# Recurrent attention and two feed-forward layers: staged loads, spare matmuls before the first tile, a new order of the first levels

## What is computed

```python
# r, k, v, w: [4, 8, 768, 48], u: [8, 48]
state = 0
for t in range(768):
    cur = einsum('bhd,bhe->bhde', u * k[t], v[t])
    y[t] = einsum('bhd,bhde->bhe', r[t], state + cur)
    state = w[t][..., None] * state + einsum('bhd,bhe->bhde', k[t], v[t])
x = y as [3072, 384]
h = x @ w_in                          # 384 x 2048
g = where(h >= 1, h, where(h <= -1, 0, (h + 1)**2 / 4))
x = g @ w_out                         # 2048 x 384
h = x @ w2_in
g = where(h > 0, h, exp(min(h, 0)) - 1)
out = g @ w2_out
```

## Time and profile before

| | us |
|---|---|
| median of 3 runs | 1023.39 (1021.88 to 1026.11) |
| the profiled execution | 1023.31 |
| its span in the profile | 1021.5 |
| TensorE (PE) busy | 989.6 (97%) |
| VectorE (DVE) busy | 554.2 (54%) |
| ScalarE (ACT) busy | 517.4 (51%) |
| GpSimd (POOL) busy | 46.7 (5%), all of it in the first 80 us |

### The profile page before, as it was taken

The page is one execution under the profiler, slowest core; times in us unless marked ns, Lnnn a source line. Parts: engine busy times, 40 slices in busy tenths (PEclk is TensorE's granted clock), DMA queues, the critical chain, the costliest instruction groups (busy, mean ns, idle before and its releaser), DMA issues.

```text
span 1021.5 us, 25102 instructions
## 1 busy us (share of the span) xinstructions
PE 989.6 (97%) x11080; PEld 812.3 (80%) x11080; DVE 554.2 (54%) x824; ACT 517.4 (51%) x926; POOL 46.7 (5%) x44
## 2 busy tenths in 40 slices
PE   4799899999999999999999999999999999999998
PEld 4788888777777777787778888888888888888886
DVE  5687877667666766776643454433433333333332
ACT  3465356454635354545456775554445444444543
POOL 5830000000000000000000000000000000000000
PEclk9899999999999999999999999999999999999999
DMA  9622032032002203020206000000000001000000
GB/s 327 200 79 96 24 121 110 3 141 78 33 28 115 80 33 115 28 80 33 95 1 216 1 31 31 32 21 11 32 31 1 31 32 31 31 1 1 31 1 31
DMA packets 24699, 61.71 MB, mean 60 GB/s; under 512 B 2448, under 2 KB 6928, under 8 KB 24592
## 3 DMA queue, kind: packets, MB, share of 16 engines
q1 hardware_dynamic: 24592, 60.12, 16.7%
HBM read 50.68 MB, written 9.44 MB: 59 GB/s over the span
## 4 chain that ended last, share of the span: by engine, by line
PE 90%; DVE 4%; POOL 2%; issue 1%; ACT 1%; DMA 1%; SPq 0%; ACTq 0%; DVEq 0%; POOLq 0%
PE down_banks L576 39%; PE up_bank L576 29%; PE g_banks L576 17%; PE y_bank L576 3%; DVE att L1025 1%; POOL win_lo L515 1%; PE y_bank L628 1%; DMA scratch<-w_in_dram 1%; PE y_bank L710 1%; POOL r_nat L525 0%; DVE r_nat L1054 0%; DVE att L1007 0%; DVE att L1037 0%; DVE ynat L1075 0%; DVE ynat L1078 0%
## 5 line engine op out<-in xcount | busy, mean ns | idle before, releaser
L576 PE MATMUL down_banks<-g_hi,wout_lo 128*128 128x512 f32 (+1 forms) x624 | 246.1, 394 | 0.0
L576 PE MATMUL down_banks<-g_hi,wout_hi 128*128 128x512 f32 (+1 forms) x624 | 235.9, 378 | 0.0
L576 PE MATMUL down_banks<-g_lo,wout_hi 128*128 128x512 f32 (+1 forms) x624 | 235.5, 377 | 0.0
L821 ACT CAST g_hi<-scratch 128x512 fp32r<-128x512 f32 (+1 forms) x192 | 116.0, 604 | 188.8 <-PE down_banks L576 118.9
L1096 DVE TENSOR_TENSOR g_lo<-scratch,g_hi 128x512 fp32r<-128x512 f32 (+1 forms) x192 | 128.4, 669 | 108.6 <-ACT g_hi L821 107.0
L576 PE MATMUL up_bank<-x_hi,win_lo 128*128 128x512 f32 (+1 forms) x480 | 182.6, 380 | 3.0 <-DVE g_lo L1096 1.8
L576 PE MATMUL up_bank<-x_lo,win_hi 128*128 128x512 f32 (+1 forms) x480 | 179.5, 374 | 0.0
L576 PE MATMUL up_bank<-x_hi,win_hi 128*128 128x512 f32 (+1 forms) x480 | 179.4, 374 | 0.0
L576 PEld LDWEIGHTS down_banks<-g_hi,wout_lo 128*128 128x128 f32 x624 | 117.8, 189 | 23.6
L576 PEld LDWEIGHTS down_banks<-g_hi,wout_hi 128*128 128x128 f32 x624 | 117.9, 189 | 23.3
L576 PEld LDWEIGHTS g_banks<-att 64*64 64x64 f32 (+1 forms) x5184 | 105.5, 136 | 36.2 <-issue 20.5
(11 more groups left out here) (98 smaller groups left out, 1075.6 us busy)
## 6 DMA issues: line engine op xcount, KB each, us to landing
att<-rT_dram SPq DMA_DIRECT2D x12, 512.0 KB, 4.0
att<-kT_dram SPq DMA_DIRECT2D x12, 512.0 KB, 5.6
att<-wT_dram SPq DMA_DIRECT2D x12, 512.0 KB, 6.5
r_nat<-rN_dram SPq DMA_DIRECT2D x12, 384.0 KB, 6.7
k_nat<-kN_dram SPq DMA_DIRECT2D x12, 384.0 KB, 7.7
att<-vN_dram SPq DMA_DIRECT2D x12, 384.0 KB, 6.9
x_dram<-r_nat SPq DMA_DIRECT2D x18, 256.0 KB, 2.3
ynat<-x_dram SPq DMA_DIRECT2D x6, 768.0 KB, 4.3
```

The lines of the kernel that those rows point to most:

```text
L576: return nc.tensor.matmul(out, lhsT, rhs, start=start, stop=stop, **kw)
L821: return nc.scalar.copy(out, in_)
```

## The change

- **Loads.** SP's first list is cut up by waits: a load is issued when an earlier one has landed (`landed(i)` waits for piece i). The order changes too: pieces 9 to 12 come before group 1's r, k and w, the others behind. Pieces 6 to 13 get buffers of their own (`extra`, `outer`), so their waits in `STAGED_BEHIND` go. The room comes from `dynamic_dma_scratch_size=2048`.
- **Spare matmuls.** `keep_busy(n)` issues n matmuls of 128x128 by 128x512 on zeros (a slice of `x_lo[1]` that DVE clears first) into `up_bank[1]`, which nothing reads: 9 before level 0, 5 after each of the levels 0 to 5, 3 after the last, and 2, 2 and 4 around the turns of x.
- **DVE.** In chunk 0, group 0 the next decays come before the mask. The mask of level 0 is for every chunk and group a product with a mask of ones and zeros (a `tensor_tensor` that writes all odd columns) in place of a predicated copy.
- **ACT.** A copy of one column at the very start has the function table loaded there. Pieces 9 to 12 are rounded where 9 to 16 were; 13 and 14 behind the rounding of x and the copy of k, the others two at a time in slots 0 to 2.
- **POOL.** Low parts 0 to 2, keys and bonus of group 0, low parts 3 to 5, the clearing of `near[1]`, low part 6, the product with v of group 0 (which no longer waits for low part 8), keys of group 1, low parts 7 to 18.
- **Diagonal.** ("values", 1, 1) moves from slot 19 to slot 21.

```diff
-                  16: [("sums", 1, 0), ("values", 1, 0)], 18: [("bonus", 1, 1), ("sums", 1, 1)], 19: [("values", 1, 1)],
+                  16: [("sums", 1, 0), ("values", 1, 0)], 18: [("bonus", 1, 1), ("sums", 1, 1)], 21: [("values", 1, 1)],
...
-STAGED_BEHIND = {**{i: 5 for i in range(9, 14)}, 18: 2, 19: 8, 20: 8, 22: 16, 23: 17, 24: 18, 25: 22, 26: 23, 27: 21}
-IDLE_PIECES = 9, 17
-PIECES_OF_SLOT = {0: (17, 18), **{f: (18 + f,) for f in range(1, 10)}}
+STAGED_BEHIND = {18: 2, 22: 16, 23: 17, 24: 18, 25: 22, 26: 23, 27: 21}
+IDLE_PIECES = 9, 13
+IDLE_AFTER_LEVEL = (5, 5, 5, 5, 5, 5, 3)
+PIECES_OF_SLOT = {0: (15, 16), 1: (17, 18), 2: (19, 20), **{f: (18 + f,) for f in range(3, 10)}}
...
             load_channels(0)
             load(masks_d, masks[:, :, :].rearrange("p l t -> p (l t)"), masks_in)
-            load_pieces(range(0, 3))
-            load_natural(0, 0)
+            load_pieces(range(0, 2))
+            sp.wait_ge(rk_in[0], 32)
+            load_pieces(range(2, 3))
+            load_natural_r(0, 0)
+            sp.wait_ge(w_in[0], 16)
+            load_natural_k(0, 0)
+            landed(0)
             load(uN, u_nat[:, :], bonus_in)
-            load_pieces(range(3, 6))
+            load_pieces(range(3, 4))
+            landed(1)
+            load_pieces(range(4, 5))
+            landed(2)
+            load_pieces(range(5, 6))
+            sp.wait_ge(nat_in[0], 32)
             load(vN[0, 0], v_[0], v_in[0])
-            load_natural(0, 1)
-            load_pieces(range(6, 9))
+            load_natural_r(0, 1)
+            landed(3)
+            load_natural_k(0, 1)
+            landed(4)
+            load_pieces(range(6, 7))
+            landed(5)
+            load_pieces(range(7, 8))
+            sp.wait_ge(v_in[0], 16)
+            load_pieces(range(8, 9))
             load(ident_d, ident[:, :], ident_in)
-            load_pieces(range(14, 19))
-            load_pieces(range(9, 14))
-            load_channels(1)
-            load_pieces(range(19, 21))
+            sp.wait_ge(nat_in[1], 32)
+            load_pieces(range(9, 12))
+            landed(6)
+            load_pieces(range(12, 13))
+            landed(7)
+            load(rT[0, 1], r_[1], rk_in[1])
+            landed(8)
+            load(kT[0, 1], k_[1], rk_in[1])
+            landed(9)
+            landed(10)
+            load(wT[0, 1], w_[1], w_in[1])
+            landed(11)
+            landed(12)
+            load_pieces(range(13, 15))
+            sp.wait_ge(rk_in[1], 32)
+            load_pieces(range(15, 17))
+            sp.wait_ge(w_in[1], 16)
+            load_pieces(range(17, 21))
...
-                pool.wait_ge(w1_lo_ready, 9 if g == 0 else 21)
+                if g == 1:
+                    pool.wait_ge(w1_lo_ready, 21)
...
-            for i in range(6):
+            for i in range(3):
                 lo_of_weights(i)
             times_keys(0)
             times_bonus(0)
+            for i in range(3, 6):
+                lo_of_weights(i)
+            pool.wait_ge(w1_lo_ready, 6)
+            nc.gpsimd.memset(near[1], 0.0).then_inc(scores_zeroed[1], 1)
+            lo_of_weights(6)
+            diagonal_output(0)
             times_keys(1)
-            for i in range(6, 9):
-                lo_of_weights(i)
-            diagonal_output(0)
-            for i in range(9, 14):
-                lo_of_weights(i)
-            pool.wait_ge(w1_lo_ready, 14)
-            nc.gpsimd.memset(near[1], 0.0).then_inc(scores_zeroed[1], 1)
-            for i in range(14, 19):
+            for i in range(7, 19):
                 lo_of_weights(i)
...
+            def keep_busy(n):
+                for _ in range(n):
+                    mm(up_bank[1][:, :], idle_work[:, 0:P], idle_work)
+            pe.wait_ge(idle_work_ready, 1)
+            keep_busy(9)
             for l in range(NL):
                 pair_products(0, 0, l)
+                keep_busy(IDLE_AFTER_LEVEL[l])
             for b in range(2):
                 attend(0, b)
             turn_k(0, 0)
-            for b in range(2):
-                turn_x(0, b)
+            keep_busy(2)
+            turn_x(0, 0)
+            keep_busy(2)
+            turn_x(0, 1)
+            keep_busy(4)
...
             act.wait_ge(consts_ready, 1)
+            copy(table_loaded[:, :], consts[:, 0:1])
...
             k_turned_of(0, 0)
+            for i in range(IDLE_PIECES[1], 15):
+                hi_of_weights(i)
...
+                if l == 0:
+                    nc.vector.tensor_tensor(
+                        near[g].rearrange("p (i t two) -> p i t two", two=2, i=2 * GP)[:, :, :, 1], products,
+                        masks[:, 0:1, :].bitcast(F32).broadcast_to([P, 2 * GP, HALF // 2]), ALU.mult).then_inc(masked[g], 1)
+                    return
...
+            nc.vector.memset(idle_work.bitcast(F32), 0.0).then_inc(idle_work_ready, 1)
             nc.vector.memset(near[0], 0.0).then_inc(scores_zeroed[0], 1)
...
                 update(0, 0, l)
+                next_decays(0, 0, l)
                 mask(0, 0, l)
-                next_decays(0, 0, l)
```

More of the change, by code:

```diff
@@ L76 @@
             W1_OUT[11:13] + W1_IN[3][2:3] + W1_OUT[13:16]
-STAGE = ["g0", "g1", "q", "scores0", "scores1", "scores2", "y0", "y1", "y2",
-         "scores_0", "scores_1", "scores_2", "scores_3", "scores_4", "v0", "v1", "state0", "state1",
+STAGE = ["g0", "g1", "q", "scores0", "scores1", "scores2", "extra0", "extra1", "extra2",
+         "outer0", "outer1", "outer2", "outer3", "outer4", "v0", "v1", "state0", "state1",
          "q", "y_0", "y_1", "keys", "state0", "state1", "q", "state0", "state1", "keys"]
-STAGED_BEHIND = {**{i: 5 for i in range(9, 14)}, 18: 2, 19: 8, 20: 8, 22: 16, 23: 17, 24: 18, 25: 22, 26: 23, 27: 21}
-IDLE_PIECES = 9, 17
-PIECES_OF_SLOT = {0: (17, 18), **{f: (18 + f,) for f in range(1, 10)}}
+STAGED_BEHIND = {18: 2, 22: 16, 23: 17, 24: 18, 25: 22, 26: 23, 27: 21}
+IDLE_PIECES = 9, 13
+IDLE_AFTER_LEVEL = (5, 5, 5, 5, 5, 5, 3)
+PIECES_OF_SLOT = {0: (15, 16), 1: (17, 18), 2: (19, 20), **{f: (18 + f,) for f in range(3, 10)}}
 F32 = mybir.dt.float32
@@ L128, in build @@
         x_lo = [sb(f"x_lo{i}", [P, KT, TOK], F32R) for i in range(2)]
+        outer = sb("outer", [P, 5, DM])
+        extra = sb("extra", [P, 3, TOK])
         scratch = sb("scratch", [P, 3, TOK])
@@ L138, in build @@
                    **{f"scores{i}": a_[1][:, i * TOK:(i + 1) * TOK] for i in range(3)},
-                   **{f"scores_{i}": a_[1][:, i * DM:(i + 1) * DM] for i in range(5)},
-                   **{f"y{i}": ynat_flat[:, i * TOK:(i + 1) * TOK] for i in range(3)},
+                   **{f"outer{i}": outer[:, i, :] for i in range(5)},
+                   **{f"extra{i}": extra[:, i, :] for i in range(3)},
                    **{f"y_{i}": ynat_flat[:, (2 + i) * DM:(3 + i) * DM] for i in range(2)},
@@ L148, in build @@
         consts = sb("consts", [P, 3])
+        table_loaded = sb("table_loaded", [P, 1])
+        idle_work = x_lo[1][:, 0, :]
         up_bank = [bank(f"up_bank{i}") for i in range(2)]
@@ L193, in build @@
         consts_ready = sem("consts_ready")
+        idle_work_ready = sem("idle_work_ready")
         scores_zeroed = [sem(f"scores_zeroed{g}") for g in range(2)]
@@ L431, in load_pieces, with landed @@
                     sp.dma_start(staged(i), src).then_inc(piece_in[STAGE[i]], 16)
+            def landed(i):
+                sp.wait_ge(piece_in[STAGE[i]], 16)
             load_channels(0)
             load(masks_d, masks[:, :, :].rearrange("p l t -> p (l t)"), masks_in)
-            load_pieces(range(0, 3))
-            load_natural(0, 0)
-            load(uN, u_nat[:, :], bonus_in)
-            load_pieces(range(3, 6))
-            load(vN[0, 0], v_[0], v_in[0])
-            load_natural(0, 1)
-            load_pieces(range(6, 9))
-            load(ident_d, ident[:, :], ident_in)
-            load_pieces(range(14, 19))
-            load_pieces(range(9, 14))
-            load_channels(1)
-            load_pieces(range(19, 21))
+            load_pieces(range(0, 2))
[5 more added lines that the diff above has]
+            landed(0)
+            load(uN, u_nat[:, :], bonus_in)
+            load_pieces(range(3, 4))
[4 more added lines that the diff above has]
+            sp.wait_ge(nat_in[0], 32)
+            load(vN[0, 0], v_[0], v_in[0])
+            load_natural_r(0, 1)
[7 more added lines that the diff above has]
+            load_pieces(range(8, 9))
+            load(ident_d, ident[:, :], ident_in)
+            sp.wait_ge(nat_in[1], 32)
[16 more added lines that the diff above has]
+            load_pieces(range(17, 21))
             sp.wait_ge(rk_multiplied[1], 1)
@@ L1210, in level_masks @@
         parts.append(mask[:, t[0] // m % 2 == 1])
-    return -np.concatenate(parts, axis=1).astype(np.int32)
+    one = np.float32(1).view(np.int32)
+    return np.concatenate([parts[0] * one] + [-p.astype(np.int32) for p in parts[1:]], axis=1).astype(np.int32)
 def channels_on_partitions(x):
@@ L1244 @@
```

(2 more changed lines are left out.)

## The result

The changed kernel took 1013.68 us (median of 6 executions, 1012.96 to 1016.68), the kernel before 1023.53 beside it (6 executions, 1021.88 to 1027.69): a ratio of 0.990 [0.988, 0.993], 9.9 us less. Forecast were 1012 us and a range of 1008 to 1020. Two more sessions gave the same changed kernel 1016.21 (ratio 0.993 [0.991, 0.995]) and 1016.82 (0.993 [0.992, 0.995]); over all its 18 executions the median is 1015.9. The gain is real and lies between 6 and 10 us.

A forecast was written before the change was run, and what follows sets the result against it. POOL's queue and the level chain, ending 0.3 us apart, bound slot 0's start, with TensorE at half clock until 41.9 us. -5.5 - 4.2 - 1.5 - 0.3 = -11.5 us from 1023.31 gave 1012; range 1008 to 1020, own range 1008.5 to 1015.

The forecast's parts named there:

- Start of slot 0: First `up` of slot 0 starts at 29.7 instead of 35.20 us: -5.5 us (-3 to -7).
- The POOL side: POOL's queue before slot 0: 3.3 us shorter, started 1.3 and 0.9 earlier, product done at 25.6, slot 0 at 29.7.
- The level side: Level chain before slot 0: 2.55 us shorter, `attend` starts at 24.7 and ends at 26.8, slot 0 at 29.7.
- the time that DVE loses beside POOL: DVE's update and decays in levels 0 and 1 beside POOL's work: 0.3 us lost, bounds 0 and 2.5.
- the level at half clock: One level at the start, with spare matmuls at half clock, costs 0.75 us.
- Slots 0 to 3: TensorE at full clock wins 3.35 and 1.5 us, DVE's pace takes back 0.6: -4.2 us, bounds 0 and -5.5.
- Mask and moved values: Level 0 mask as a product, felt in slots 5, 14, 26: -1.5 us; values moved two slots on: -0.3.
- Two signs: Before slot 0 no level longer than 3.0 us; an ACT wait for a DMA in slots 0 to 2 would disprove.
- Rival 1: TensorE's clock falls again in slots 0 to 3, losing 1.5 us and another 1.5: 1015 us; chance 0.16.
- Rival 2: SP's loads are throttled too far, and waits for landings eat 4 us: 1016 us; chance 0.11.
- Rival 3: Spare matmuls before slot 0 never raise the clock, levels last 4.1 us, slot 0 at 41.5: 1028 us; chance 0.10.
- Rival 4: DVE stands behind POOL at every chance, the gap from `attend` to `up` doesn't shrink: 1020 us; chance 0.06.

The follow-up runs named there:

- the spares in slot 17: Changed kernel with seven more spare matmuls in slot 17, between the waits for the masks and the output: 1017.01 us, ratio 0.994; its profiled execution took 1021.25.
- the POOL experiment: Changed kernel with POOL's first low part held back until DVE has made the decays of level 1: 1015.96 us, ratio 0.992.
- the last kernel: Changed kernel with three, four and seven more spare matmuls in slots 1, 2 and 17, and POOL held back behind level 1's decays: 1014.18 us, ratio 0.992.

## Why the prediction was right, and where its terms were off

The time, 1013.68, lies 1.7 us over the forecast and inside its own range (1008.5 to 1015); the medians of the later sessions, 1016.2 and 1016.8, lie beyond that, within the whole range. The closeness to 1012 is in part luck: the session of the result had few falls of the clock, and over all 18 executions the median is 3.9 over the forecast. The mechanism came as told: pair products of 1.14, slots 0 to 3 at 1.00, the mask at 0.68, the last stage moved as a block. Of the forecast sum of -11.5 us the profiled execution gave -10.1. Some errors inside the sum cancelled.

**Start of slot 0: -4.4, forecast -5.5.** The POOL side held in its sum: its product was done at 26.1 for 25.6. POOL began 2.43 us earlier (9.11 for 11.54), where 1.28 + 0.9 had been taken off. Its queue up to the end of the product got 2.5 us shorter and not 3.3: the first three low parts took 5.46 us beside DVE, and the product waited 0.36 for the sums. That wait ties the two chains together, since DVE makes the sums behind the levels; the prediction didn't count it. It was 1.25 us with all loads at once, 3.05 without spares and 4.07 in the bad execution of the spares in slot 17.

The level side was too short. `attend` started at 25.36 for 24.7, out of three terms: the time that DVE loses beside POOL was 1.35 us (1.62 - 1.23 and 1.58 - 0.63), not 0.3; an "issue" stall of 0.41 was not foreseen; and the level at half clock, counted with 0.75, did not come (in the other two executions level 0 took 1.46 and 1.39 us, and level 1 began no later). By the rule of the Trainium skill, "SBUF — State Buffer", "Who interferes with whom", 1.9 us had been worked out. The measurement is nearer to the rule than to my value, and the update and decays of the POOL experiment, back at 1.23 and 0.63, agree with it. The prediction said that this would cost only 0.6 us, the level chain having a microsecond to spare. By its own sum there was nothing to spare, for both chains ended at 29.7; the 1.9 us would have given slot 0 at 31.3.

The last 0.5 us lies behind `attend`: from its end at 27.43 to `up` are 3.35 us where I took 2.85. I had the second batch's output begin when `attend` ends. DVE begins the first output only behind its update, at 26.68, and the second at 27.86, 0.43 us behind `attend`; its four output instructions end at 29.01. The second turn starts at 29.12, so the spares around the turns are almost wholly under them, although the chain of waits runs through them.

**Slots 0 to 3: -4.66, forecast -4.2.** Inside its bounds; slots 1 and 2 are indeed DVE's, with TensorE waiting 0.57 and 1.27 us. What the slots win is the full clock: their pair products take 1.14 us. That the spares bring it there isn't shown: the traced execution without spares won 4.3 us in these slots, and the one with the spares alone, where the clock was down in slots 1 and 2, won 2.5. What the spares are needed for in the traces is the levels, that is, the start of slot 0.

**Mask and moved values: -1.0, forecast -1.8.** The mask's own term was right: 0.53 us came by slot 7, 0.56 by slot 16 and 0.56 by slot 28, 1.65 for 1.5, and with the predicated mask all three stay away. The moved values gave 0.15 by slot 21 and took 0.27 by slot 25. Another 0.43 went between slots 9 and 10, to the "issue" gap of 0.36 at 64.92; the kernel before has none there. It isn't DVE's doing, although an update just before took 1.99 us beside POOL's low parts: TensorE's wait for `g_lo` in slot 9 is 0.33 for 0.30 before. Nothing later than slot 28 changed. Neither part alone can be seen in the kernel's time.

**Two signs went against the prediction.** It wanted no level longer than 3.0 us: from level 0 to 1 took 3.24, from 2 to 3 3.88, from 4 to 5 3.10. And it named an ACT wait for a load in slots 0 to 2: ACT stood 1.48 us for a piece of w_out until 32.10, ahead of slot 0's activation. That cost nothing, for the third execution of the changed kernel has no such wait and wins the same 4.66 us in slots 0 to 3.

**The rivals.** Rival 1 put the danger in the wrong place. The clock held in slots 0 to 3 of the three traced executions of the changed kernel; it fell, in two of them, at 16 to 20 us behind the 1.39 us gap (0.4 us on slot 0) and in the 2.1 us wait of slot 17 (2.4 us), which the prediction never looked at although the kernel before has it too (2.09 us at 111.46). Over all the profiles that have this wait without spares in it, the kernel before among them, the clock fell in six of twelve. This is most of the distance between 1013.7 and 1016.5. Of the changed kernel's 18 executions the 7 with a mean granted clock of 0.997 or more took 1012.96 to 1015.68 (median 1013.5), the other 11 took 1015.16 to 1020.73 (median 1016.7). Five of the 7 are of the session of the result.

Rival 2 had the wrong sign: with the loads unthrottled the kernel took 2.4 to 5.5 us more. In the traced execution 1.7 us of that lie at slot 0; the rest are falls of the clock, of which the one in slot 17 comes in the changed kernel too. The Trainium skill, "DMA: Bandwidth & Descriptors", section "Anatomy of one DMA", which the prediction sets beside the 2.9 us of the earlier trace rows, is about loads that GpSimd issues; this one was issued from SP, so only the number agrees. Rival 3 fell with the first pair product. Rival 4's mechanism (DVE behind POOL) was there, with 1.35 us of price.

**Parts don't add up.** The spares alone give 0. Taking one part out costs, against 1013.7 and against 1016.8 (the lowest and highest of the changed kernel's medians; it didn't run in the session of three of these): the spares 7.1 or 4.0 us, the spares between levels and turns 5.6 or 2.5 (3.1 against the changed kernel beside it), the throttled loads 5.5 or 2.4, POOL's queue 6.0 or 2.9. The spares, the loads and the queue make 18.6 or 9.3 together, more than the 9.9 or 6.2 us of the whole change. These medians hold different numbers of falls of the clock. Among the traced executions whose record shows no fall, taking out the spares cost 5.2 us (1018.40 for 1013.22) and POOL's queue 3.4. Two chains end within about half a microsecond of each other, and shortening one alone leaves the other: with the spares alone POOL ends at 30.5; without them the levels put slot 0 at 35.57; with POOL held back 1.5 us are won on the levels and POOL's product, 0.8 later, takes them back.

**The "issue" stalls.** By their times they are waits for TensorE's own program. They come at fixed places. Counted in matmuls they end at the 351st (between the first and the second spare of level 4), the 477th, 730th, 982nd or 1486th, and one of 0.14 us at the 223rd. The kernels without spares between the levels have none at these places. Each ends 1.3 to 1.6 us after a 16 KB packet on the instruction queue was through, in all 20 cases; in the two further executions of the changed kernel the packet was through more than 1.9 us before the 351st, and there is no stall. At the 351st the two kernels whose loads aren't throttled had 2.26 and 1.33 us; of the nine profiles with throttled loads and these spares three had none, four 0.39 to 0.49, one 1.22 and one 2.23. So the packets come late under either order of loads, and that throttling helps them is likely from these counts and not shown. The gap of 0.35 to 0.37 us at 64.92, which ten profiles have in the same piece of the program, has no packet just ahead of it and stays unexplained.

**What stays open.** Why the clock falls behind the same gap in one execution and not in the next, and what brought it up ahead of slot 0 without spares. That the filled gaps of the last kernel bring the time down is likely and not shown.

## What to carry to other kernels

When two chains end together, cut both in one change and judge neither part by itself: here the spares alone gave nothing, and all the rest without them 2 us. In this kernel nine spares at the start alone didn't keep TensorE's clock up through the levels; spares in every gap did in most executions. Once the clock is high the long single waits of later stages are worth a look, since what one of them costs (2.4 us here) differs between executions and hides as noise. One traced execution is one draw: look where its time lies before a part's worth is read from it. Before moving POOL's work earlier, look at what DVE does in SBUF at that time.

## What the runs showed that was not expected

- With nine spares at the start and none behind, the clock went from 1.00 to 0.50 inside a gap of 1.82 us and stayed there from 7.7 to 31.6 us; gaps of 1.39 and 2.10 us were passed at full clock in one execution and not in others.
- Without any spare one execution was at full clock from slot 0 on.
- TensorE stood still for 0.4 to 2.3 us, marked "issue", between two spare matmuls of level 4, in eight of eleven profiles, and went on 1.3 to 1.5 us after a 16 KB packet of instructions. Shorter stalls of the same kind came at four later places.
- DVE and POOL both lose when they meet: 1.35 us of DVE's time over one update and its decays, and 1.7 us of POOL's over three low parts.
- A predicated copy took 1.34 us where the product with a mask, over the same elements, took 0.68.
